# Sharing out the rational gate's quotient between VectorE, GpSimd and PSUM in the first step of a fused attention and two-FFN kernel

## What is computed

```
qn = q / (norm(q) + 1e-6)         # norms over the tokens, likewise kn from k
s  = kn^T @ qn / tau              # 256 x 256
a  = softmax(s);  x = v @ a       # N x 256
h  = x @ w_in                     # N x 2048
P  = a0 + a1 h + a2 h^2 + a3 h^3
Q  = 1 + |b0||h| + |b1| h^2
y  = (P / (Q + 1e-6)) @ w_out     # N x 256
u  = y @ w_in2
out = (u * clip(u + 3, 0, 6) / 6) @ w_out2
```

## Time and profile before

| | |
|---|---|
| median of 3 runs | 1125.63 us (1124.23 to 1125.67) |
| the profiled execution, device time | 1124.4 us |
| its span, first to last instruction | 1122.6 us |
| TensorE busy | 1097.7 us (98%) |
| VectorE busy | 901.0 us (80%) |
| ScalarE busy | 868.9 us (77%) |
| GpSimd busy | 781.2 us (70%) |
| mean granted TensorE clock | 0.995 of full speed |

### The profile page before, as it was taken

One profiled execution on the slowest core, in us unless ns is written; L12 is line 12 of the kernel. 1 busy time (PEld: TensorE's weight loads), 2 busy tenths in 40 slices (PEclk: granted clock), 3 DMA queues, 4 the chain that ended last, 5 costly groups with the idle time before them and its releaser, 6 DMA issues.

```text
span 1122.6 us, 16081 instructions
## 1 busy us (share of the span) xinstructions
PE 1097.7 (98%) x5004; PEld 921.3 (82%) x5004; DVE 901.0 (80%) x1286; ACT 868.9 (77%) x1468; POOL 781.2 (70%) x625
## 2 busy tenths in 40 slices
PE   9978799999999999999999999999999999999998
PEld 8877688888888888888888888888888888888887
DVE  6689999987887887887897888788798788787632
ACT  6698888877877877787887777877777787777643
POOL 0278889777776777776777776777777677776643
PEclk9999899999999999999999999999999999999999
DMA  9931010010010020020020020010011010010010
GB/s 351 294 128 20 0 20 1 15 19 1 10 30 1 0 39 1 0 38 0 0 38 0 1 38 0 0 32 6 1 22 17 1 20 1 1 20 1 1 19 20
DMA packets 105465, 33.82 MB, mean 30 GB/s; under 512 B 92982, under 2 KB 98742, under 8 KB 105398
## 3 DMA queue, kind: packets, MB, share of 16 engines
q1 hardware_dynamic: 104832, 32.52, 11.6%
q10 hardware_dynamic: 566, 0.52, 0.1%
HBM read 26.87 MB, written 6.16 MB: 29 GB/s over the span
## 4 chain that ended last, share of the span: by engine, by line
PE 91%; DVE 5%; ACT 1%; issue 1%; DMA 0%; POOL 0%; SPq 0%; DVEq 0%; ACTq 0%
PE H L447 15%; PE H L448 14%; PE H L449 14%; PE YP L449 7%; PE YP L448 7%; PE YP L447 7%; PE OP L449 7%; PE OP L448 7%; PE OP L447 7%; PE OP L480 3%; DVE SQ L926 1%; DVE H L911 1%; DVE g_hi L919 1%; DVE T L904 1%; PE OP L618 1%
## 5 line engine op out<-in xcount | busy, mean ns | idle before, releaser
L401 POOL TENSOR_TENSOR SQ<-SQ,AB 128x512 f32<-128x512 f32 (+1 forms) x192 | 247.6, 1290 | 256.4 <-ACT SQ L721 256.0
L415 POOL TENSOR_TENSOR g_lo<-R,g_hi 128x512 fp32r<-128x512 f32 (+1 forms) x191 | 243.4, 1274 | 28.8 <-ACT g_hi L753 28.8
L407 POOL TENSOR_TENSOR g_lo<-SQ,Y 128x512 fp32r<-128x512 f32 (+1 forms) x192 | 244.7, 1274 | 6.2 <-DVE SQ L934 6.2
L719 ACT ACTIVATE AB<-H,absb 128x512 f32<-128x512 f32 (+1 forms) x192 | 130.4, 679 | 144.9 <-PE H L449 144.9
L904 DVE TENSOR_TENSOR T<-T,H 128x512 f32<-128x512 f32 (+1 forms) x192 | 128.9, 672 | 85.4 <-ACT T L727 85.4
L919 DVE SCALAR_TENSOR_TENSOR g_hi<-H,coef,Y 128x512 fp32r<-128x512 f32 (+1 forms) x192 | 141.6, 737 | 53.7 <-ACT Y L740 51.3
L447 PE MATMUL H<-vT_hi,wf_hi 128*128 128x512 f32 (+1 forms) x384 | 150.3, 392 | 14.6 <-DVE wf_lo L891 8.8
L926 DVE SCALAR_TENSOR_TENSOR SQ<-SQ,g_hi 128x512 f32<-128x512 f32 (+1 forms) x192 | 155.7, 811 | 6.6
L940 DVE SCALAR_TENSOR_TENSOR R<-R,H 128x512 f32<-128x512 f32 (+1 forms) x192 | 128.1, 667 | 35.2 <-ACT R L746 35.2
L746 ACT ACTIVATE R<-H 128x512 f32<-128x512 f32 (+1 forms) x192 | 113.4, 591 | 51.7 <-PE H L449 50.9
L447 PE MATMUL YP<-g_hi,wd_hi 128*128 128x512 f32 (+1 forms) x384 | 149.6, 390 | 3.5 <-POOL g_lo L407 3.3
(11 more groups left out here) (104 smaller groups left out, 2054.0 us busy)
## 6 DMA issues: line engine op xcount, KB each, us to landing
qk<-in_q SPq DMA_DIRECT2D x22, 256.0 KB, 5.2
qk<-in_k SPq DMA_DIRECT2D x22, 256.0 KB, 6.1
v_blocks<-in_v SPq DMA_DIRECT2D x88, 64.0 KB, 2.3
out<-o_tok SPq DMA_DIRECT2D x80, 64.0 KB, 1.9
wd_raw<-in_moe_w_out SPq DMA_DIRECT2D x8, 512.0 KB, 9.2
w_raw_a<-in_moe_w_in SPq DMA_DIRECT2D x2, 1024.0 KB, 10.7
wu_raw<-in_moe_w_in SPq DMA_DIRECT2D x4, 512.0 KB, 6.2
qk<-in_q SPq DMA_DIRECT2D x3, 128.0 KB, 3.0
```

What stands on the lines that cost most here:

```text
L401: nc.gpsimd.tensor_tensor(SQ[:, j % 4, 0:w], SQ[:, j % 4, 0:w], AB[:, j % 2, 0:w], ALU.add)\
L407: nc.gpsimd.tensor_tensor(g1_lo[:, j % 4, 0:w], SQ[:, j % 4, 0:w], Y[:, j % 2, 0:w], ALU.mult)\
L415: nc.gpsimd.tensor_tensor(g2_lo[:, j % 4, 0:w], R[:, j % 2, 0:w], g2_hi[:, j % 4, 0:w].bitcast(fp32), ALU.subtract).then_inc(g2_lo_done, 1)
```

## The change

All of it lies in the first step, but for the slots of `V_AT`. In step 0 ScalarE writes |b0||h| not into `AB` but into the second bank of `OP`; VectorE (`q_sum_0`), not GpSimd, adds up Q, the constant included, from `SQ` and that bank; GpSimd (`product_0`), not VectorE, makes the product Q * g1_hi; and `rest` and `quotient_lo` run two slots behind h in place of one. From piece 1 on the fold puts both halves into the first bank of `OP`, and each engine waits for both halves. Weight splits and the transposes of v are put at other slots.

```diff
+    LAG_REST_0 = 2
-    V_AT = 5, 8
+    V_AT = 6, 10
-    WU2_AT = 2, 6, 10, 11, 12, 13, 15, 23
-    WD2_AT = 14, 16, 17, 18, 19, 27, 29, 30
+    WU2_AT = 3, 5, 7, 8, 9, 12, 15, 17
+    WD2_AT = 11, 14, 16, 18, 19, 27, 29, 30
...
+        def folded(n, c):
+            w = PIECES[n] * P
+            return OP[:, 0, c * w:(c + 1) * w] if n >= 1 else OP[:, c, 0:w]
...
+            def product_0(j):
+                w = width(0)
+                wait_chunk(pool, g1_hi_done, (0, j))
+                nc.gpsimd.tensor_tensor(SQ[:, j % 4, 0:w], SQ[:, j % 4, 0:w], g1_hi[:, j % 4, 0:w].bitcast(fp32),
+                                        ALU.mult).then_inc(product_done, 1)
...  GpSimd's step
+                    at = slot(t, j)
+                    if at is not None and 0 <= at - LAG_REST_0 < J:
+                        quotient_lo(0, at - LAG_REST_0)
+                    if at is not None and 0 <= at - LAG_DIVIDE < J:
+                        product_0(at - LAG_DIVIDE)
-                    if exists(t):
+                    if exists(t) and not first:
                         q_body(t, j)
...  TensorE's fold
+                if n >= 1:
+                    pe.wait_ge(fold_lo, CT * n)
...  ScalarE's q_terms
+                if isinstance(t, int) and t == 0:
+                    if j >= 1:
+                        wait_chunk(act, w_done, (0, j - 1))
+                    term = OP[:, 1, 0:w]
+                else:
+                    wait_chunk(act, w_done, back(t, j, 2))
+                    term = AB[:, j % 2, 0:w]
+                nc.scalar.activation(term, h, ACT.Abs, scale=absb[:, 0:1])
...  VectorE
+            def q_sum_0(j):
+                w = width(0)
+                wait_chunk(dve, q_done, (0, j))
+                nc.vector.scalar_tensor_tensor(SQ[:, j % 4, 0:w], SQ[:, j % 4, 0:w], Q_CONST, OP[:, 1, 0:w],
+                                               ALU.add, ALU.add).then_inc(w_done, 1)
...  VectorE's step
+                    if at is not None and 0 <= at - LAG_REST_0 < J:
+                        rest(0, at - LAG_REST_0)
+                    if first and j - 1 in PIECE_AT[:-1]:
+                        fold_split(PIECE_AT.index(j - 1) + 1)
...
                     if x := stage(t, j - LAG_DIVIDE):
                         quotient_hi(*x)
-                        product(*x)
-                        rest(*x)
+                        if at is None or at >= J + LAG_DIVIDE:
+                            product(*x)
+                            rest(*x)
+                    if first:
+                        q_sum_0(j)
```

More of the change, by code:

```diff
@@ L75, in attention_ffn_ffn @@
     assert tiles_of[-1] == BT
-    assert sum(PIECES) == J and J // 2 in PIECE_AT
+    assert sum(PIECES) == J and J // 2 in PIECE_AT and CT * max(PIECES) * P == 512
     QUARTER, UNIT = J * C // 4, J * C // 8
@@ L423, in step @@
             def step(t, par):
+                first = isinstance(t, int) and t == 0
                 for j in range(J):
-                    if exists(t):
+                    at = slot(t, j)
[4 more added lines that the diff above has]
+                    if exists(t) and not first:
                         q_body(t, j)
@@ L436, in step @@
                         wd2_split(WD2_AT.index(slot(t, j)))
-                    if y := stage(t, j - LAG_DIVIDE):
-                        quotient_lo(*y)
+                    if at is None or at >= J + LAG_DIVIDE:
+                        if y := stage(t, j - LAG_DIVIDE):
+                            quotient_lo(*y)
             every_step(pool, step)
@@ L513, in fold @@
                     pe.wait_ge(w1_in[PIECE_AT[n] // (J // 2)], 16)
+                if n >= 1:
+                    pe.wait_ge(fold_lo, CT * n)
                 for c in range(CT):
-                    if n >= 1:
-                        pe.wait_ge(fold_lo, CT * (n - 1) + c + 1)
-                    else:
+                    if n == 0:
                         pe.wait_ge(probT_ready, c + 1)
                     for d in range(CT):
-                        done = nc.tensor.matmul(OP[:, c, 0:PIECES[n] * P], probT[:, d, c * P:(c + 1) * P],
+                        done = nc.tensor.matmul(folded(n, c), probT[:, d, c * P:(c + 1) * P],
                                                 w_raw_a[:, d, cols],
```

17 lines of the change are left out of this document (7 added, 10 removed).

## The result

The kernel before took 1125.28 us (median of 6 runs, 1124.23 to 1125.67), the changed kernel 1118.2 us (median of 6, 1117.61 to 1118.82): a ratio of 0.9942, with an interval of 0.9932 to 0.9951. That is 5.5 to 7.7 us faster. The forecast was 1122.0 with a range down to 1119.0, so the direction was right, the size too small, and the time lies outside the range. The trace of the first profiled execution spans 1117.0 us (its own time 1118.82).

What follows compares the result with a forecast made beforehand. The bound was when TensorE's closed row begins, with VectorE pacing step 0. Last sum 2.5 us earlier plus a hand-over 1.1 shorter gave 3.6 us: 1125.6 - 3.6 = 1122.0 us, range 1119.0 to 1125.8.

Steps and rivals of the forecast that it cites:

- GpSimd's lateness: Step 0, behind the splits at slots 3, 7, 11 and 14: product_0 late by 0.35 to 0.4 us each, 1.5 us.
- slots 2 to 15, first 14 links of the sum: Step 0 from q_sum_0(1) at 60.81: fourteen slots of 2.70 to 3.70 us added up to 45.1 us.
- hand-over to `up1(1, 2)`: From q_sum_0(15) to step 1's up1(1, 2): 10.2 us in place of 11.3, 1.1 shorter; bounds 0 and 2.3.
- What bounds it: TensorE's matmuls from 145 us on run closed; only an earlier start of up1(1, 2), at 121.19 us, moves the end.
- VectorE's instructions: Step 0: five per slot, one dependent link left, 2.70 us in place of 3.14; q_sum_0 takes 0.62 us.
- The loop through ScalarE: Step 0: root, its square, Abs, Square, q_sum_0 and back to root take 2.72 us; 2.74 taken per slot.
- The cover of `V_AT`: Later v transposes cost nothing: v's split is needed only next step; without that room one transposition, 0.70 us, would show.
- The splits' table: New weight-split slots cost nothing: splits all made earlier than their users or where they were.
- The fold's bank: Fold in a single bank costs nothing: TensorE's new wait for both halves is already met by up1 of that slot.
- The clock: Half clock (1.2 GHz) at up1(1, 2) stays, since the idle stretch before it stays near 5 us; its end moves along.
- more is saved: Rival, 0.15: GpSimd never late (+1.5) and up1(1, 2) at full clock (+1.3); gain 5.1 to 6.4, 1119.2 to 1120.5 us.
- The slower rival: Rival, 0.13: GpSimd becomes the bound, product_0 late behind each of 11 splits in step 0; 1128.2 to 1130.4 us.

Runs made afterwards that it cites:

- second profile of after: The same changed kernel profiled a second time, nothing altered, without the low-clock stretch in step 0: span 1115.8 us, its own time 1117.65 us.
- a_vat_old: Changed kernel with the old slots of v (V_AT = 5, 8) put back, everything else as changed: 1120.39 us, ratio 0.9963 to the kernel before.
- a_q10: Changed kernel with the sum of step 1's chunk 0 also on VectorE, its term in the free OP bank: 1116.31 us, ratio 0.9929 to the kernel before.
- a_lag1: Changed kernel with rest and quotient_lo one slot behind h in place of two (LAG_REST_0 = 1): 1130.51 us, ratio 1.0051 to the kernel before.
- b_splits: Kernel before with only the new weight-split slots (WU2_AT, WD2_AT): 1126.22 us against 1124.42, ratio 1.0016.
- b_order: Kernel before with only step 0's new order, product still on VectorE, sum on GpSimd ahead of quotient_lo: 1131.47 us against 1124.42, ratio 1.0062.
- a_term_sbuf: Changed kernel with the sum's term |b0||h| written to AB in SBUF as before: 1121.14 us, ratio 0.9969 to the kernel before.

## Why the prediction was wrong, step by step

The path was right and two terms were not. The prediction put GpSimd's lateness behind four splits at 1.5 us, and none came before the last sum. It put `V_AT` at nothing, and in step 1 alone that is 0.75 us. The rest, 0.6 us, are slots and a hand-over taken a little too long.

In the forecast's own counting, absolute starts in the second profile of after against those of the earlier trace rows:

| step | forecast | measured |
|---|---|---|
| slots 2 to 15, first 14 links of the sum | 45.1 | 105.40 - 60.75 = 44.65 |
| GpSimd late behind four splits | 1.5 | 0.0 by `q_sum_0(15)`, 0.2 behind it |
| `q_sum_0(15)` starts | 107.4 | 105.40 (first profile 106.57) |
| hand-over to `up1(1, 2)` | 10.2 | 10.07 |
| `up1(1, 2)` earlier by | 3.6 | 5.72 |
| `V_AT` in step 1 (on the count) | 0 | 0.73 to 0.77 |

- **What bounds it** was right: the end moved with the start of the closed row, and nothing behind 145 us changed.
- **VectorE's instructions** were right in the link (2.70 from `rest` to `rest`; from sum to sum the slots 2, 14 and 15 take 2.80 to 2.83) and too dear in the duration: 0.54 to 0.555 for the sum in place of 0.62. I had taken L934's, "since its kinds of operands are the same", but L934 reads PSUM as its first input and the sum reads it as its second. The row of that kind stood in the earlier trace rows: L904, `T<-T,H`, reads `H` in PSUM second and takes 0.55, so it isn't so that all instructions that read `H` take 0.62. The rule of the Trainium skill, "VectorE: DVE Perf Modes", section on the TRN2 errata, on PSUM's fixed term doesn't show in this place of the operand: the sum takes no longer than L926's shortest, 0.557. It would not have moved the slot either way.
- **The loop through ScalarE** held: measured slots without a fold or a transposition are 2.63 to 2.89 us, with a fold 3.41 to 3.73, with a transposition 3.22 and 3.40. The fourteen came in 0.45 us under the sum, through slots 7 and 11, the fold slots right behind a transposition: 3.41 each in place of 3.70. The term into PSUM takes 0.54 us against the 0.56 of L719, inside its bound and on the side that the Trainium skill, "ScalarE: Activation LUTs", section "Step-by-step: what each stage is for", names: it calls PSUM the faster destination.
- **GpSimd's lateness was the first step that failed**: 1.5 us put in, none found. The arithmetic was a slot's length against GpSimd's work in that slot (3.28 against 2.78, less some overlap), and it left out that GpSimd comes into such a slot ahead. Its own waits in step 0 (second profile) are the reserve: four times for `rest`, 4.5 us in all, and four times for `quotient_hi`, 1.0 us in all. A lump behind such a wait is taken up by it. In slot 4 `product_0(3)` ends at 70.38 + 1.02 = 71.40, and VectorE asks for it at 71.44. The fit is that close, and `a_vat_old` shows the price of missing it: 1.15 us in one slot behind two splits.
- **The cover of `V_AT` was the second**, "TensorE doesn't wait there in any step". The rows said otherwise: of the two waits for L934 I took the one of 5.1 us and left the other, 0.6 us, out. It was the transposition of slot 21, with `product` pushed into GpSimd's sum behind it. I had even priced it, "without that room one transposition, 0.70 us, would show"; measured 0.75. And in step 0 I asked only whether v's transposition has room until its user, not what its split meets on GpSimd where it stands. That is the 1.83 us that `V_AT` decides there in the changed kernel, the same cover as in the point above, seen from the other side: the two tables interlock, and I had priced them one by one.
- **The splits' table** "costs nothing": alone it costs 1.8 us in the kernel before, through `product`, and it is worth 1.2 in the changed one. The sum was hardly hurt by it, since the forecast's slots were built with the new table; as a sentence it was wrong.
- **The fold's bank** at nothing and the **hand-over** at 10.2 were right, the second in part also in its cause (`a_q10`: 1.34 us of it hang on GpSimd's queue).
- **The clock** was right where I left it in: half clock behind a wait of 4.5 us, worth 1.0 when filled. The other low stretch, in the middle of step 0, I had not foreseen; it is the difference between the two profiles.
- **The rival "more is saved"** (1119.2 to 1120.5) named the first failing step, GpSimd never late, and its 1.5 us; together with the 0.75 of step 1, which no rival held, and the 0.45 of the slots it comes to what was measured: 3.6 + 1.5 + 0.45 + 0.13 (hand-over) + 0.75 = 6.43, against 6.45. Its other half, the full clock for `up1(1, 2)`, didn't come. The slower rival's mechanism exists (`a_lag1`, 12 us), but the second slot of lag removes it.

What stays open: the last 0.5 us of `V_AT` in step 0 of the changed kernel, why the three `V_AT` variants of the old one gain so differently there, and what decides whether the clock falls in step 0. Each part was tested by itself or taken back by itself; their sizes overlap and don't add up to the whole.

## What to carry to other kernels

When a waits row says "2 times" and the longest is not the total, find the other one: it stood at the very slot whose cover the argument needed. Where an engine has lumps (a split here, a transposition there), don't price each against the length of a slot; lay the tables over each other, and give each slot at most one lump, with the engine's own waits in the slots before as its reserve. A table that costs 1.8 us in one kernel can bring 1.2 in the next, so time such a table in the kernel that it is meant for. And where a VectorE instruction with two SBUF inputs runs beside a busy GpSimd, ask first whether one of them can come from PSUM: taking that back cost 3.5 of 6.45 us here, while the order alone brought 1. For its price, take the row with the same kinds of operands in the same places.

## What the hardware showed that was not expected

- A VectorE instruction with its first input in SBUF and its second in PSUM took 0.54 to 0.555 us for 384 columns, sixteen times, beside GpSimd work of 86% of the time. The same with both in SBUF took 0.546 to 1.412. The one with PSUM as its first input and SBUF as its second, `rest`, took 0.61 to 0.62.
- A VectorE instruction caught in this way behaved as if it began its work only when GpSimd's ended: of those on 384 columns that took over 0.7 us (six in before, nine in `b_splits`, fifteen in `b_order`, nine in `a_term_sbuf`) all but one ended 0.40 to 0.43 us after the GpSimd instruction that ran when it started, whether it had started 0.02 or 0.7 us behind it. The one left started just as one GpSimd instruction followed on another. On 512 columns the one of slot 21 (before) took 1.77 us and ended 0.54 after. GpSimd's splits also fell from 1488 to 1284 ns when nothing of the kind ran beside them.
- TensorE's granted clock was 0.61 and 0.53 in the two windows from 66 to 70 us in one execution of a program and not in another, with its busy time alike (3.72 and 3.64 us of those 4). With ScalarE at 97% that cost the kernel 1.25 us.
- A float32 matmul of 128 columns stands in the trace as two rows, and takes 0.22 us in a row of 34.
